# Attention's matrix powers and its inverse on TensorE: products that use the same weights joined to 128 columns, in quarters

## The chip, the cores and the metric

The kernel runs on one core of a Trainium2 chip. The metric is the device time of one execution in microseconds. A core has a matmul engine (TensorE, PE in the profile, with PEld for its weight loads), three engines for elementwise work (VectorE or DVE, ScalarE or ACT, GpSimd or POOL) and SyncE (SP), which issues DMAs. Matmul results land in PSUM, from which DVE and ACT copy them to SBUF. Each engine works through its own queue in order; semaphores tie them together.

## What is computed

The whole program is an attention with a state per head, then a mixture of experts, then a feed-forward layer. The change is in the attention alone:

```python
batch, n_heads, seq, head_dim = (4, 8, 768, 40)
for t in range(S):
    y[:, :, t] = np.einsum('bhd,bhde->bhe', rt, state)
    Sa = np.einsum('bhde,bhe->bhd', state, at)
    state_decay = state * wt[:, :, None, :] - np.einsum('bhd,bhe->bhde', Sa, bt)
    state = state_decay + np.einsum('bhd,bhe->bhde', vt, kt)
```

The 768 steps are cut into 12 chunks of 64. Inside a chunk the dependence of a step on the earlier ones is a triangular 64x64 matrix, whose inverse the kernel builds; from chunk to chunk a state is carried.

## The kernel before

`attention` handles the 32 heads in 8 groups of 4, each with 12 chunks, so a "wide" product covers a half of the chunks (6) for four heads: 24 matmuls of 64x64x64, written as `square` (L365). The inverse of `I + N` is a product of `I + N^(2^k)`: `n2`, `n4`, `n8`, `n16` are powers of N, `t2`, `t4`, `t8` the same powers of its transpose (a power of one kind takes the other as weights, so both are kept), and `w2`, `w4`, `w8`, `w16` multiply the inverse so far, `wb`, by `n2`, `n4`, ... and add. `_0` and `_1` are the halves. Note that `t4` and `w2` both load `n2` as weights, and `t8` and `w4` both load `n4`.

Each wide product goes into one of three PSUM slots (`wide0` to `wide2`), by its number modulo 3. Product n may start when product n-3 has been taken:

```python
if n >= 3 and kind != "Y":
    taken(pe, *in_order[n - 3])
```

`n`, `t`, `K`, `B`, `V`, `L`, `UT`, `ST` and `X` are taken by ACT (`BY_ACT`), the others by DVE. `w` products are added to `wb` by DVE (L641).

Alongside runs the recurrence over the chunks of the group before, in hops `u`, `s`, `r`: a small product on PE, then a copy of it on ACT (`u`, L553), the state on DVE (`s`, L681) or the right-hand side on DVE (`r`, L674), and the next hop waits for that.

The order is written out by hand. One table, `ORDER`, holds the tokens of a turn of the loop (a turn prepares one group and runs the recurrence of the one before); PE, ACT and DVE each walk through the same table and do their share, in that order. `LEAD` is the table of the first turn (turn 0), which has no recurrence, and turns 1 to 7 use `ORDER`. `p0` and `p1` are tokens of DVE alone: `make_decays` (L661) for the next group, with two scans (L664, L667) and two short steps, in turns 0 to 6. GpSimd rounds N, starts `wb` (L352), subtracts the identity (L356), and scales the operands of the next group.

Of the kernel before, what the change touches and what calls it, by code (L numbers as in the profile page):

```python
# [27 lines left out]
P = 128  # L28
# [8 lines left out]

ORDER = """u ST1 N0 s UT1 T0 r N1 u H1 I1 t2_0 s J1 Y1 r T1 u n2_0 s t2_1 r w2_0 u K1 s n2_1 r t4_0 u p0 t4_1 K0 n4_1 s  # L40
n4_0 M0 B0 r w4_0 u w2_1 ST0 s M1 r UT0 w4_1 u n8_0 s t8_1 r n8_1 u t8_0 V1 p1 s n16_1 n16_0 w8_0 X1 r H0 u
w16_0 s w8_1 I0 r E0 B1 u w16_1 L0 s V0 r E1 u J0 s Y0 L1 r F0 X0 F1 u""".split()

LEAD = """N0 K1 N1 K0 T0 M1 T1 n2_0 M0 n2_1 B0 t2_0 t2_1 w2_1 n4_0 w2_0 B1 n4_1 p0 t4_1 t4_0 V1 n8_0 w4_0 t8_1 t8_0 p1
w8_0 n8_1 n16_0 w4_1 n16_1 w16_0 w8_1 V0 L0 w16_1 E0 E1 L1 F0 F1""".split()
DRAIN = """u s ST1 r u s r u UT1 s r H1 u s r u s r u s r u s I1 r J1 Y1 u UT0 s r H0 u X1 s r u ST0 s I0 r J0 Y0 u s
X0 r u""".split()
CHAIN = ("u", "s", "r")
FIRST_HALF = ("UT0", "ST0", "H0", "I0", "J0", "Y0", "X0")
SECOND_HALF = ("ST1", "UT1", "H1", "I1", "J1", "Y1", "X1")  # L50
BY_ACT = ("n2", "n4", "n8", "n16", "t2", "t4", "t8", "K", "B", "V", "L", "UT", "ST", "X")


def split(tok):
# [10 lines left out]
def attention(nc, wdec, at, kb, vt, vd, rb, rc, gate_w, x, logits, ident):  # L65

    GR, _, D, _, S = at.shape
    C = 64
# [21 lines left out]
    for it in range(GR + 2):  # L90
        for tok in order_of(it):
            g = group_of(tok, it)
            if g is None or tok in CHAIN or tok[0] in "Jp":
                continue
            by = "act" if split(tok)[0] in BY_ACT else "dve"
            ends[by] += 1
            number[tok, g] = len(number)
            count[tok, g] = by, ends[by]
    in_order = list(number)

    def chunk_of(hop):
# [3 lines left out]
    with ExitStack() as ctx:  # L105
# [24 lines left out]
        tpow = [sb(f"tpow{b}", [P, 2, S], BF16) for b in range(2)]  # L130
        wb = sb("wb", [P, 2, S], BF16)
# [31 lines left out]

        def taken(eng, tok, g):

            by, n = count[tok, g]
            eng.wait_ge(act_done if by == "act" else dve_done, n)

        def cells():

# [193 lines left out]
        def _(pe):  # L364
# [8 lines left out]
            def wide(tok, g):  # L373
# [29 lines left out]
                elif kind[0] in "nt":  # L403
                    p = int(kind[1:])
                    at_ = (p.bit_length()) % 2
                    if p == 2:
                        pe.wait_ge(rounded, 2 * g + half + 1)
                        taken(pe, f"T{half}", g)
                    else:
                        taken(pe, f"n{p // 2}_{half}", g)  # L410
                        taken(pe, f"t{p // 2}_{half}", g)
                    left, right = (tpow, npow) if kind[0] == "n" else (npow, tpow)
                    m = square(half, out, left[at_], right[at_])
                elif kind[0] == "w":
                    p = int(kind[1:])
                    taken(pe, f"n{p}_{half}", g)
                    if p == 2:
                        pe.wait_ge(started, 2 * g + half + 1)
                    else:
                        taken(pe, f"w{p // 2}_{half}", g)  # L420
# [130 lines left out]
        def _(act):  # L551
# [3 lines left out]
            def take(tok, g):  # L555
# [6 lines left out]
                if kind[0] in "nt":  # L562
                    p = int(kind[1:])
                    dst = (npow if kind[0] == "n" else tpow)[(p.bit_length() + 1) % 2]
                    if kind == "t4":
                        act.wait_ge(started, 2 * g + half + 1)
                    m = copy(dst[:, :, at_], t[:, :, 0:W])
                elif kind in ("K", "B"):
                    m = copy(kbtok[b2][:, 0 if kind == "K" else 1, half * HC:half * HC + HC].rearrange("q (b c) h d -> q b (c h) d", b=2),
                             t[:, :, 0:W].rearrange("q b (n f) -> q b n f", f=C)[:, :, :, 0:D])  # L570
# [23 lines left out]
            for it in range(GR + 2):  # L594
                hop = 0
                for tok in order_of(it):
# [3 lines left out]
                    if tok in CHAIN:  # L600
# [8 lines left out]
                        elif kind == "r" and c < NC - 1:  # L609
# [4 lines left out]
                    elif tok[0] not in "Jp" and split(tok)[0] in BY_ACT:  # L614
                        take(tok, g)
                    elif tok in ("w16_0", "w16_1"):
                        half = split(tok)[1]
                        taken(act, tok, g)
                        copy(wb[:, :, cols(half, W)], w0[g % 2][:, :, cols(half, W)]).then_inc(w_rounded, 1)

        @block.vector
        def _(dve):
# [3 lines left out]
            def take(tok, g):  # L626
# [771 lines left out]
```

## Time and profile before

| | us |
|---|---|
| median of 3 runs | 1591.04 (1590.13 to 1598.68) |
| profiled execution | 1593.16 |
| its span, first to last instruction | 1591.4 |
| PE busy | 1440.8 (91%) |
| DVE busy | 578.8 (36%) |
| ACT busy | 587.5 (37%) |
| GpSimd busy | 293.0 (18%) |

Times are those of one profiled execution. An engine's queue is read from top to bottom: when its next instruction waits, all behind it wait. Attention lies between about 28 and 576 us. The timeline merges instructions of a line that follow each other; "x24" with 0.57 us is a product of 24 matmuls from its first start to its last end. A matmul of a float32 operand stands as two instructions.

### The profile page before, as it was taken

Reading aid. Unit: us, or ns where it says so; the run is one execution under the profiler, and the core shown is the slowest. Engines: PE = TensorE matmul, PEld = TensorE weight load, DVE = VectorE, ACT = ScalarE, POOL = GpSimd, SP = SyncE. Lnnn points to the kernel's source line nnn. Section 1 sums busy time; section 2 is a strip of 40 time slices with the busy share of each in tenths; the row PEclk is TensorE's granted clock in tenths of the full one; section 3 lists DMA queues with packets and bytes.
Section 4 is the critical chain, followed back from the end, with each engine's and each line's share of the span. In section 5 each row is a group of like instructions: output and inputs, shape, how many; then the busy total and the mean of one; then the engine's idle time right before and its main releaser. Section 6 shows DMA issues by size and latency. Waiting matters only on the chain.

```text
span 1591.4 us, 45341 instructions
## 1 busy us (share of the span) xinstructions
PE 1440.8 (91%) x19945; PEld 1115.7 (70%) x19945; DVE 578.8 (36%) x1107; ACT 587.5 (37%) x1167; POOL 293.0 (18%) x263
## 2 busy tenths in 40 slices
PE   2889989899898727999999999999699999999999
PEld 2778878788787626888888888888435555555556
DVE  6665565564643260000000000000165445445441
ACT  1555364453544321111211112111176545554451
POOL 5532233232220001111111111111320010000000
PEclk9787797876878657999999999999799999999999
DMA  3223232222311177555555555556410011000000
GB/s 117 61 87 94 68 105 74 80 82 73 92 44 35 52 228 248 185 170 172 168 181 183 170 170 168 185 178 203 128 50 21 26 32 31 25 17 9 13 9 21
DMA packets 87553, 161.20 MB, mean 101 GB/s; under 512 B 39552, under 2 KB 53888, under 8 KB 87360
## 3 DMA queue, kind: packets, MB, share of 16 engines
q1 hardware_dynamic: 79776, 132.41, 26.5%
q0 software_dynamic: 7584, 25.90, 5.3%
q8 instruction: 160, 2.62, 0.7%
q14 instruction: 33, 0.27, 0.1%
HBM read 141.39 MB, written 16.88 MB: 99 GB/s over the span
## 4 chain that ended last, share of the span: by engine, by line
PE 60%; DMA 1%; issue 1%; DVE 0%; ACT 0%; POOL 0%; POOLq 0%; DVEq 0%
PE pY L1027 15%; PE pY L1169 13%; PE pH L1008 13%; PE pH L1156 11%; PE pH L1013 4%; PE pH L1159 3%; PE pX L997 1%; PE pX L1144 1%; PE pX L998 0%; DMA xs<-x,slot_token 0%; DMA rows<-results,pos 0%; POOL rows L1135 0%; DVE down L1244 0%; DMA results<-ys 0%; ACT mxT L1198 0%
## 5 line engine op out<-in xcount | busy, mean ns | idle before, releaser
L1027 PE MATMUL pY<-down,hT 128*128 x880 | 245.9, 433 | 0.0
L1008 PEld LDWEIGHTS pH<-exT,up 128*128 128x128 f32 x1760 | 207.9, 194 | 11.5 <-issue 1.7
L1053 ACT ACTIVATE hT<-pH 128x512 f32<-128x512 f32 x110 | 59.7, 594 | 419.4 <-PE pH L1013 419.4
L1061 DVE COPY ys<-pY 128x320 f32<-128x320 f32 x55 | 27.0, 492 | 507.1 <-PE pY L1027 507.1
L1008 PE MATMUL pH<-exT,up 128*128 128x128 f32 x1760 | 208.5, 277 | 2.5 <-ACT exT L1046 2.5
L1169 PE MATMUL pY<-wout,down 128*128 128x320 f32 x768 | 210.4, 433 | 0.0
L1027 PEld LDWEIGHTS pY<-down,hT 128*128 128x128 f32 x880 | 163.0, 190 | 61.2
L1169 PEld LDWEIGHTS pY<-wout,down 128*128 128x128 f32 x768 | 144.3, 190 | 60.7 <-issue 3.0
L1156 PE MATMUL pH<-mxT,win 128*128 128x512 f32 x384 | 172.5, 603 | 4.9 <-ACT mxT L1198 4.7
L1156 PEld LDWEIGHTS pH<-mxT,win 128*128 128x128 f32 x384 | 73.8, 193 | 91.6 <-issue 82.2
L988 POOL DMA_DIRECT2D results<-ys x55 | 31.9, 580 | 428.4 <-DVE ys L1061 428.4
L1135 POOL DMA_INDIRECT rows<-results,pos x48 | 45.7, 952 | 221.4 <-DVE mix L1223 209.9
L1206 ACT ACTIVATE down<-down 128x512 f32<-128x512 f32 x64 | 39.9, 629 | 122.0 <-DVE down L1244 122.0
L553 ACT ACTIVATE npow<-wide 128x768 bf16<-128x768 f32 x80 | 63.3, 811 | 39.6 <-PE wide L427 23.1
L553 ACT ACTIVATE uv<-chain 64x80 f32<-64x80 f32 x192 | 44.3, 231 | 84.6 <-PE chain L525 82.9
L1235 DVE TENSOR_TENSOR down<-down 128x512 f32<-128x512 f32 x64 | 40.0, 686 | 94.6 <-ACT down L1212 94.5
L1245 DVE COPY down<-pH 128x512 f32<-128x512 f32 x96 | 65.2, 679 | 0.0
L1013 PE MATMUL pH<-exT,up_rest 64*128 64x128 f32 x880 | 63.9, 285 | 0.0
L202 POOL TENSOR_TENSOR kbT<-kbT,after 128x1536 f32<-128x1536 f32 x15 | 51.6, 3444 | 62.5 <-DMA kbT<-in_kb 62.5
L979 POOL DMA_INDIRECT xs<-x,slot_token x55 | 53.8, 978 | 49.8 <-POOLq L732 30.1
L525 PE MATMUL chain<-rhs,w 64*64 64x40 f32 x768 | 49.1, 250 | 10.7 <-DVE rhs L674 5.0
L1244 DVE TENSOR_SCALAR down<-pH 128x512 f32<-128x512 f32 x64 | 43.7, 683 | 39.8 <-PE pH L1159 31.0
(189 smaller groups left out, 2146.0 us busy)
## 6 DMA issues: line engine op xcount, KB each, us to landing
up<-in_moe_w SPq DMA_DIRECT2D x55, 1024.0 KB, 5.2
up_rest<-in_moe_w SPq DMA_DIRECT2D x110, 128.0 KB, 5.1
down<-in_moe_w SPq DMA_DIRECT2D x8, 1280.0 KB, 14.3
results<-ys POOLq DMA_DIRECT2D x55, 160.0 KB
wfr<-in_wdec SPq DMA_DIRECT2D x32, 240.0 KB
kbT<-in_kb SPq DMA_DIRECT2D x32, 240.0 KB
uv<-in_vt SPq DMA_DIRECT2D x16, 312.0 KB, 3.8
aT<-in_at SPq DMA_DIRECT2D x16, 240.0 KB
```

What stands on the lines that cost most here:

```text
L202: unit.tensor_tensor(kbT[:, i], kbT[:, i], backwards, ALU.mult).then_inc(kb_scaled, 1)
L525: m = pe.matmul(chain[x:x + 64, h, 64:64 + D], w0[b2][x:x + 64, h, cols(c, C)], rhs[b2][x:x + 64, h, c, :], start=True, stop=True)
L553: return nc.scalar.activation(out, in_, ACT.Copy, scale=scale)
L979: nc.gpsimd.indirect_dma_start(out=xs[t % 3][:], out_offset=None, in_=x, in_offset=bass.IndirectOffsetOnAxis(ap=slot_token[:, t:t + 1], ax ...
L1008: pe.matmul(pH[t % 2][b][:, c, :], up[t % NU][:, k, f * P:(f + 1) * P], xT[t % 2][:, k, :], start=(c == 0 and k == 0), stop=False, skip_gr ...
L1013: m = pe.matmul(pH[t % 2][b][:, c, :], up_rest[t % NU][at, c * P:(c + 1) * P], xT[t % 2][at, 2, :], start=False, stop=True, skip_group_che ...
L1027: m = pe.matmul(pY[t % 2][:, 0:D], hT[t % 2][:, j, :], down[:, bass.ds(e, 1), j, :].rearrange("q n d -> q (n d)"), start=(j == 0), stop=(j ...
L1053: nc.scalar.activation(hT[t % 2][:, b * HT:(b + 1) * HT, :], pH[t % 2][b][:], ACT.Relu).then_inc(h_copied[b], 1)
L1156: pe.matmul(pH[f % 4], win[:, k, f * P:(f + 1) * P], xT[g % 2][:, k, :], start=(k == 0), stop=False)
L1159: pe.matmul(pH[f % 4], win_rest[at, f // 2 * P:(f // 2 + 1) * P], xT[g % 2][at, 2, :], start=False, stop=True).then_inc(h_done, 1)
L1169: m = pe.matmul(pY[t % 2][:, 0:D], h[g % 2][:, f, j * P:(j + 1) * P], wout[:, f, :], start=(f == 0), stop=(f == FT - 1))
L1245: nc.vector.tensor_copy(h[g % 2][:, GT * q + f, :], pH[f]).then_inc(h_used, 1)
```

## The change

`t4` and `w2` become `q4`, `t8` and `w4` become `q8`. A `q` product loads a block of `n2` (or `n4`) once and multiplies it by 128 columns, 64 of `t` and 64 of `wb`, which therefore lie in one tensor `tw`. Its results have twice the columns, so one slot holds a quarter of the chunks: `q4_0` to `q4_3` and `q8_0` to `q8_3` replace the eight half products, in eight places of the tables that these had. A quarter is 12 matmuls. ACT copies its `t` part and then DVE adds its `w` part; a slot is free when both are through. `q` products therefore stand in the queues of both ACT and DVE.

```diff
-ORDER = """u ST1 N0 s UT1 T0 r N1 u H1 I1 t2_0 s J1 Y1 r T1 u n2_0 s t2_1 r w2_0 u K1 s n2_1 r t4_0 u p0 t4_1 K0 n4_1 s
-n4_0 M0 B0 r w4_0 u w2_1 ST0 s M1 r UT0 w4_1 u n8_0 s t8_1 r n8_1 u t8_0 V1 p1 s n16_1 n16_0 w8_0 X1 r H0 u
+ORDER = """u ST1 N0 s UT1 T0 r N1 u H1 I1 t2_0 s J1 Y1 r T1 u n2_0 s t2_1 r q4_0 u K1 s n2_1 r q4_1 u p0 q4_2 K0 n4_1 s
+n4_0 M0 B0 r q8_0 u q4_3 ST0 s M1 r UT0 q8_2 u n8_0 s q8_3 r n8_1 u q8_1 V1 p1 s n16_1 n16_0 w8_0 X1 r H0 u
...
-LEAD = """N0 K1 N1 K0 T0 M1 T1 n2_0 M0 n2_1 B0 t2_0 t2_1 w2_1 n4_0 w2_0 B1 n4_1 p0 t4_1 t4_0 V1 n8_0 w4_0 t8_1 t8_0 p1
-w8_0 n8_1 n16_0 w4_1 n16_1 w16_0 w8_1 V0 L0 w16_1 E0 E1 L1 F0 F1""".split()
+LEAD = """N0 K1 N1 K0 T0 M1 T1 n2_0 M0 n2_1 B0 t2_0 t2_1 q4_2 n4_0 q4_0 B1 n4_1 p0 q4_3 q4_1 V1 n8_0 q8_0 q8_2 q8_1 q8_3
+p1 w8_0 n8_1 n16_0 n16_1 w16_0 w8_1 V0 L0 w16_1 E0 E1 L1 F0 F1""".split()
...
-BY_ACT = ("n2", "n4", "n8", "n16", "t2", "t4", "t8", "K", "B", "V", "L", "UT", "ST", "X")
+BY_ACT = ("n2", "n4", "n8", "n16", "t2", "K", "B", "V", "L", "UT", "ST", "X")
...
+        def together(kind):
+
+            return (1, 1, 0) if kind == "q4" else (0, 0, 1)
...
+                elif kind[0] == "q":
+
+                    p = int(kind[1:]) // 2
+                    taken(pe, f"n{p}_{half // 2}", g)
+                    if p == 2:
+                        taken(pe, f"t2_{half // 2}", g)
+                        pe.wait_ge(started, 2 * g + half // 2 + 1)
+                    else:
+                        taken(pe, f"q4_{half}", g)
+                    lo = together(kind)[0]
+                    for c in range(HC // 2):
+                        k = half * (HC // 2) + c
+                        for i, h, e, x, z in cells():
+                            m = pe.matmul(out[x:x + 64, h, cols(c, 2 * C)], npow[(p.bit_length() + 1) % 2][x:x + 64, h, cols(k, C)],
+                                          tw[x:x + 64, lo:lo + 2, h, cols(k, C)], start=True, stop=True)
...
+                elif kind[0] == "q":
+                    if kind == "q4":
+                        act.wait_ge(started, 2 * g + half // 2 + 1)
+                    m = copy(by_chunk(tpow[0 if kind == "q4" else 1][:, :, cols(half, W // 2)]),
+                             t[:, :, 0:W].rearrange("q h (c s f) -> q h c s f", s=2, f=C)[:, :, :, together(kind)[1], :])
...
-                elif kind in ("w2", "w4", "w8"):
+                elif kind[0] == "q":
+
+                    dve.wait_ge(act_done, count[tok, g][0][1])
+                    part = by_chunk(wb[:, :, cols(half, W // 2)])
+                    m = nc.vector.tensor_tensor(part, t.rearrange("q h (c s f) -> q h c s f", s=2, f=C)[:, :, :, together(kind)[2], :], part, ALU.add)
+                elif kind == "w8":
```

DVE's queue around `p0` in turn 1 (`p0` is the four rows from `after` to `dec_0`; `wb` or `tw` with 192 is a `w` add, `st` the state of hop `s`, `rhs` that of hop `r`, `mT` is `M0`). Before:

```order
L674 TENSOR_TENSOR rhs<-chain,rhs 128x2x40
L664 SCALAR_TENSOR_TENSOR after<-wfr,mark_r 128x768
L665 TENSOR_TENSOR fend<-after,wfr 128x12
L666 RECIPROCAL mark<-fend 128x12
L667 SCALAR_TENSOR_TENSOR dec_0<-wfr,mark 128x768
L681 SCALAR_TENSOR_TENSOR st<-chain,fend,fs 128x40 x2
L639 TENSOR_TENSOR mT<-wide,mask_u 128x2x384
```

Now, in the same place:

```order
L711 TENSOR_TENSOR rhs<-chain,rhs 128x2x40
L676 TENSOR_TENSOR tw<-wide,tw 128x2x192
L701 SCALAR_TENSOR_TENSOR after<-wfr,mark_r 128x768
L702 TENSOR_TENSOR fend<-after,wfr 128x12
L703 RECIPROCAL mark<-fend 128x12
L704 SCALAR_TENSOR_TENSOR dec_0<-wfr,mark 128x768
L676 TENSOR_TENSOR tw<-wide,tw 128x2x192
L718 SCALAR_TENSOR_TENSOR st<-chain,fend,fs 128x40 x2
L671 TENSOR_TENSOR mT<-wide,mask_u 128x2x384
```

An add (of `q4_1`) now stands ahead of `p0`, and one (of `q4_2`) between `p0` and the state.

PE's queue in the same place, from `t4_1` to `w4_0`, with the slot's number in `wide0` to `wide2`. Before:

```order
L369 MATMUL wide0<-tpow1,npow1 64x64 x24
L395 MATMUL wide1<-ident,kbT 128x128 x6
L369 MATMUL wide2<-npow1,tpow1 64x64 x24
L532 MATMUL chain<-uv0,kbtok0 40x40 x4
L369 MATMUL wide0<-npow1,tpow1 64x64 x24
L390 MATMUL wide1<-aT1,kbT 64x64 x24
L395 MATMUL wide2<-ident,kbT 128x128 x6
L514 MATMUL chain<-st,aT0 64x40 x4
L369 MATMUL wide0<-wb,npow0 64x64 x24
```

Now:

```order
L441 MATMUL wide0<-tw,npow1 64x128 x12
L406 MATMUL wide1<-ident,kbT 128x128 x6
L380 MATMUL wide2<-npow1,tw 64x64 x24
L561 MATMUL chain<-uv0,kbtok0 40x40 x4
L380 MATMUL wide0<-npow1,tw 64x64 x24
L401 MATMUL wide1<-aT1,kbT 64x64 x24
L406 MATMUL wide2<-ident,kbT 128x128 x6
L543 MATMUL chain<-st,aT0 64x40 x4
L441 MATMUL wide0<-tw,npow0 64x128 x12
```

Nothing moved here; the first row, which is `q4_2` now, and the fifth, `n4_0`, share slot `wide0` as `t4_1` and `n4_0` did, and the first is now freed by ACT and DVE instead of ACT alone.

DVE's queue around `p1` in turn 1 (the four rows from `after` to `dec_1`). Before:

```order
L641 TENSOR_TENSOR wb<-wide,wb 128x2x384
L681 SCALAR_TENSOR_TENSOR st<-chain,fend,fs 128x40 x2
L674 TENSOR_TENSOR rhs<-chain,rhs 128x2x40
L664 SCALAR_TENSOR_TENSOR after<-wfr,mark_r 128x768
L665 TENSOR_TENSOR fend<-after,wfr 128x12
L666 RECIPROCAL mark<-fend 128x12
L667 SCALAR_TENSOR_TENSOR dec_1<-wfr,mark 128x768
L681 SCALAR_TENSOR_TENSOR st<-chain,fend,fs 128x40 x2
L641 TENSOR_TENSOR wb<-wide,wb 128x2x384
```

Now:

```order
L676 TENSOR_TENSOR tw<-wide,tw 128x2x192
L718 SCALAR_TENSOR_TENSOR st<-chain,fend,fs 128x40 x2
L676 TENSOR_TENSOR tw<-wide,tw 128x2x192
L711 TENSOR_TENSOR rhs<-chain,rhs 128x2x40
L676 TENSOR_TENSOR tw<-wide,tw 128x2x192
L701 SCALAR_TENSOR_TENSOR after<-wfr,mark_r 128x768
L702 TENSOR_TENSOR fend<-after,wfr 128x12
L703 RECIPROCAL mark<-fend 128x12
L704 SCALAR_TENSOR_TENSOR dec_1<-wfr,mark 128x768
L718 SCALAR_TENSOR_TENSOR st<-chain,fend,fs 128x40 x2
L678 TENSOR_TENSOR tw<-wide,tw 128x2x384
```

The adds of `q8_3` and `q8_1` are new, one ahead of hop `r`'s step and one ahead of `p1`.

## Rows read from the trace of the kernel before

**Rows 1.** The page's first lines: span, busy time and share of each engine.
```profile
span 1591.4 us, 45341 instructions
PE 1440.8 (91%) x19945; PEld 1115.7 (70%) x19945; DVE 578.8 (36%) x1107; ACT 587.5 (37%) x1167; POOL 293.0 (18%) x263
```

**Rows 2.** Attention's stretch: PE, PEld, DVE, ACT, POOL busy, granted clock, DMA share, GB/s.
```profile
60.00:560.00 500.00, 442.89 (x13867) 399.24 (x13866) 269.76 (x498) 237.18 (x618) 126.28 (x68) 0.79 0.26 73
```

**Rows 3.** PE's waits in that stretch: us in total, times, longest.
```profile
PE chain L532 <- ACT uv L553: 8.1, 24, 0.7
...
PE wide L369 <- issue: 5.6, 7, 1.9
PE wide L434 <- issue: 5.4, 7, 2.2
```

**Rows 4.** Timeline of turn 3, DVE's `p0` and what follows; ACT's taking of `t4_0`.
```profile
207.62 2.93 DVE L664 TENSOR_TENSOR_SCAN after<-wfr,mark_r 128x768 f32<-128x768 f32 x1
...
211.06 1.76 DVE L667 TENSOR_TENSOR_SCAN dec<-wfr,mark 128x768 f32<-128x768 f32 x1
212.73 0.40 DVE L681 SCALAR_TENSOR_TENSOR st<-chain,fend,fs 128x40 f32<-128x40 f32 x2
...
208.23 0.80 ACT L553 ACTIVATE tpow<-wide 128x768 bf16<-128x768 f32 x1
```

**Rows 5.** Timeline of turn 3, PE: `t4_1`, `s`, `n4_0`, `B0`, `r`.
```profile
208.01 0.61 PE L369 MATMUL wide<-tpow,npow 64*64 64x64 bf16 x24
...
209.85 0.35 PE L532 MATMUL chain<-uv,kbtok 128*40 128x40 f32 x8
210.27 0.57 PE L369 MATMUL wide<-npow,tpow 64*64 64x64 bf16 x24
...
211.59 0.88 PE L395 MATMUL wide<-ident,kbT 128*128 128x128 f32 x6
213.19 0.33 PE L514 MATMUL chain<-st,aT 40*64 40x40 f32 x8 [0.72 <-DVE st L681]
```

**Rows 6.** Groups by shape: takes of 384 and of 768 elements a partition.
```profile
L553 ACT ACTIVATE uvT<-wide 104x384 f32<-104x384 f32 x32 | 13.9, 488 | 20.2 <-PE wide L447 20.2
...
L650 DVE TENSOR_TENSOR yT<-wide,dec 128x384 f32<-128x384 f32 x32 | 16.4, 553 | 41.4 <-PE wide L485 41.4
...
L553 ACT ACTIVATE tpow<-wide 128x768 bf16<-128x768 f32 x48 | 38.5, 809 | 22.1 <-PE wide L369 21.3
...
L641 DVE TENSOR_TENSOR wb<-wide,wb 128x768 bf16<-128x768 f32 x48 | 45.7, 954 | 18.5 <-PE wide L369 17.4
```

**Rows 7.** Timeline of turn 3: GpSimd's subtraction, and DVE from `p1` on.
```profile
205.35 3.58 POOL L356 TENSOR_TENSOR n<-n,eye 128x768 f32<-128x768 f32 x2
...
220.61 1.75 DVE L664 TENSOR_TENSOR_SCAN after<-wfr,mark_r 128x768 f32<-128x768 f32 x1
...
224.54 0.40 DVE L681 SCALAR_TENSOR_TENSOR st<-chain,fend,fs 128x40 f32<-128x40 f32 x2
225.91 0.96 DVE L641 TENSOR_TENSOR wb<-wide,wb 128x768 bf16<-128x768 f32 x1 [0.97 <-PE wide L369]
228.55 0.24 DVE L674 TENSOR_TENSOR rhs<-chain,rhs 128x80 f32<-128x80 f32 x1 [1.68 <-PE chain L514]
```

**Rows 8.** Timeline of turn 3, ACT: the copy of hop `u` after `UT0`, and `t8_0`.
```profile
218.57 0.47 ACT L553 ACTIVATE uv<-chain 64x80 f32<-64x80 f32 x2
...
222.99 0.81 ACT L553 ACTIVATE tpow<-wide 128x768 bf16<-128x768 f32 x1
```

**Rows 9.** The lead: DVE's `p0` and `w8_0`, PE's `w4_1`, then a window (columns as rows 2).
```profile
45.80 1.75 DVE L664 TENSOR_TENSOR_SCAN after<-wfr,mark_r 128x768 f32<-128x768 f32 x1
...
55.57 0.93 DVE L641 TENSOR_TENSOR wb<-wide,wb 128x768 bf16<-128x768 f32 x1
56.55 0.85 PE L369 MATMUL wide<-wb,npow 64*64 64x64 bf16 x24 [3.42 <-DVE wb L641]
...
56.50:66.00 9.50, 9.39 (x333) 9.27 (x334) 5.31 (x6) 4.09 (x6) 7.93 (x3) 0.50 0.01 3
```

**Rows 10.** The page's row on the queue that brings instructions: packets, MB, share.
```profile
q8 instruction: 160, 2.62, 0.7%
```

More of the change, by code:

```diff
@@ L94, in attention @@
                 continue
-            by = "act" if split(tok)[0] in BY_ACT else "dve"
-            ends[by] += 1
             number[tok, g] = len(number)
-            count[tok, g] = by, ends[by]
+            count[tok, g] = []
+            for by in ("act", "dve") if tok[0] == "q" else ("act",) if split(tok)[0] in BY_ACT else ("dve",):
+                ends[by] += 1
+                count[tok, g].append((by, ends[by]))
     in_order = list(number)
@@ L129, in attention @@
         npow = [sb(f"npow{b}", [P, 2, S], BF16) for b in range(2)]
-        tpow = [sb(f"tpow{b}", [P, 2, S], BF16) for b in range(2)]
-        wb = sb("wb", [P, 2, S], BF16)
+        tw = sb("tw", [P, 3, 2, S], BF16)
+        tpow, wb = [tw[:, 0], tw[:, 2]], tw[:, 1]
         w0 = [sb(f"w0{b}", [P, 2, S]) for b in range(2)]
@@ L164, in taken, with taken_half @@
         def taken(eng, tok, g):
-            by, n = count[tok, g]
-            eng.wait_ge(act_done if by == "act" else dve_done, n)
+            for by, n in count[tok, g]:
+                eng.wait_ge(act_done if by == "act" else dve_done, n)
+        def taken_half(eng, kind, half, g):
+            for quarter in (2 * half, 2 * half + 1):
+                taken(eng, f"{kind}_{quarter}", g)
+        def together(kind):
+            return (1, 1, 0) if kind == "q4" else (0, 0, 1)
         def cells():
@@ L410, in wide @@
                         taken(pe, f"n{p // 2}_{half}", g)
-                        taken(pe, f"t{p // 2}_{half}", g)
+                        if p == 4:
+                            taken(pe, f"t2_{half}", g)
+                        else:
+                            taken_half(pe, f"q{p // 2}", half, g)
                     left, right = (tpow, npow) if kind[0] == "n" else (npow, tpow)
                     m = square(half, out, left[at_], right[at_])
+                elif kind[0] == "q":
[4 more added lines that the diff above has]
+                        pe.wait_ge(started, 2 * g + half // 2 + 1)
+                    else:
+                        taken(pe, f"q4_{half}", g)
[5 more added lines that the diff above has]
+                                          tw[x:x + 64, lo:lo + 2, h, cols(k, C)], start=True, stop=True)
                 elif kind[0] == "w":
@@ L416, in wide @@
                     taken(pe, f"n{p}_{half}", g)
-                    if p == 2:
-                        pe.wait_ge(started, 2 * g + half + 1)
+                    if p == 8:
+                        taken_half(pe, "q8", half, g)
                     else:
-                        taken(pe, f"w{p // 2}_{half}", g)
+                        taken(pe, f"w8_{half}", g)
                     m = square(half, out, npow[(p.bit_length() + 1) % 2], wb)
@@ L564, in take @@
                     dst = (npow if kind[0] == "n" else tpow)[(p.bit_length() + 1) % 2]
-                    if kind == "t4":
-                        act.wait_ge(started, 2 * g + half + 1)
                     m = copy(dst[:, :, at_], t[:, :, 0:W])
+                elif kind[0] == "q":
[3 more added lines that the diff above has]
+                             t[:, :, 0:W].rearrange("q h (c s f) -> q h c s f", s=2, f=C)[:, :, :, together(kind)[1], :])
                 elif kind in ("K", "B"):
@@ L613, in _ @@
                             m.then_inc(fs_ready, 1)
-                    elif tok[0] not in "Jp" and split(tok)[0] in BY_ACT:
+                    elif tok[0] == "q" or tok[0] not in "Jp" and split(tok)[0] in BY_ACT:
                         take(tok, g)
```

## The prediction

> **What bounds the kernel now.** I read the page first: TensorE (PE) is busy 91% of a span of 1591.4 us [rows 1]. The change touches only attention, some 560 us of it, so the next view is the busy time of that stretch: from 60 to 560 us PE is busy for 442.9 of 500 us at a mean granted clock of 0.79 [rows 2]. PE takes its work in one fixed order, so what counts is where PE stands still, and the view of who waited for whom tells that: its idle time is many short waits, on the recurrence's copies (8.1 us in 24 waits, none over 0.7) and on nothing the profile shows ("issue": 5.6 us before the squares and 5.4 before another line, up to 2.2 us each) [rows 3]. No wait is long because each thing that PE needs is taken off early enough. The question is whether the new order of takers keeps that.
>
> The timeline of one steady turn (turn 3 of the loop) shows the place where it is tight. At 207.62 VectorE (DVE) starts `p0`, the decays of the next group: a scan of 2.93 us, two short steps and a scan of 1.76 us. Its next work, the state of hop `s`, starts at 212.73 [rows 4]. For 5.1 us nothing that DVE takes from PSUM is taken. Yet PE runs on through `t4_1`, `K0`, `n4_1`, `s`, `n4_0`, `M0` and `B0` and idles only 0.72 us, before hop `r` at 213.19 [rows 5], because `t4_1`, `K0`, `n4_1` and `n4_0` are all taken by ScalarE (ACT).
>
> **The change part by part.**
>
> *The product.* A half product of 24 matmuls at the full clock lasts 0.57 us [rows 5]; less the 0.19 us of the last one, 16.5 ns from one to the next. They alternate between two halves of the array, so each half spends 33 ns on 64 columns, which are 26.7 ns at 2.4 GHz: 6.3 ns are not columns. No row shows a bf16 product of 64 rows with 128 columns. Joining a `t` half and a `w` half takes 24 loads away. If a matmul of 128 columns keeps one such 6.3 ns, the pair saves 12 x 6.3 = 0.075 us; if it keeps none, 0.15 us. Below these, nothing is saved: in the lead, at 1.2 GHz, the product of 24 took 0.85 us [rows 9], 26.5 ns each or 53 per half of the array, which is 64 columns and nothing else. I take 0.11 us x 4 pairs x 8 groups = 3.5 us at the full clock, and as PE often waits there anyway, -2 us.
>
> *A rule against this.* The row says 33 ns per 64 columns in each half of the array. The Trainium skill (TensorE: Matmul & The Clock Gate, Back-to-back issue gap) gives about 60 cycles for a matmul of up to 64 columns and 134 for one of 128, so a joined matmul would be longer than two small ones, by 14 cycles. By that a joined pair of products would cost 0.07 us more, and the term would be +2 us and not -2. The trace disagrees at 64 columns (33 ns against 25), which is where the saving would come from.
>
> *The instruction stream.* 768 matmuls and 768 weight loads go, of 13867 + 13866 in the 500 us [rows 2], 5.5%. The kernel's stream came in 160 blocks [rows 10]. If the stream's arrival set PE's pace everywhere, 5.5% of 500 us, 27 us, would go; if it set none, nothing. The "issue" waits say it sets some: eleven rows of that kind hold about 25 us, and 5.6 us stand before the squares [rows 3]. I take -1 us per turn, -7 us, and keep 0 and -20 for the range. The trace has waits of up to 2.2 us for nothing shown, on a stream that doesn't branch. The Trainium skill (Runtime: NRT & Kernel Launch, Instruction fetch mechanics) says that crossing a block is mostly hidden; by it this term would be 0 and the sum 7 us higher.
>
> *The takers.* Before, a product has one taker: 0.81 us on ACT or 0.95 us on DVE. A quarter now has two, one after the other, since DVE waits for ACT. No row shows 128x384 taken with this pattern; the nearest are 0.49 us on ACT and 0.55 us on DVE [rows 6]. So a slot is held 0.49 + 0.05 + 0.55 = 1.1 us. The engines have room (270 and 237 us busy of 500, [rows 2]); what matters is who stands in line.
>
> *p0, the main term.* `q4_1` stands where `t4_0` stood, but DVE must take it before it starts `p0`. ACT took `t4_0` at 208.23 [rows 4]; so DVE is through with `q4_1` at 208.23 + 1.1 = 209.3 and starts `p0` 1.7 us later than now. Part comes back: the first scan took 2.93 us beside GpSimd's subtraction, which lasts to 208.93, against 1.75 us in `p1`, where the whole block of decays lasted 3.9 us [rows 4, 7]. So `p0` now ends at 213.3. Behind it on DVE stands `q4_2`, which PE fills just before `K0`, and its add ends at 213.8. Three products later `n4_0` writes the same slot, and PE may not start it before that. It started at 210.27; `M0`, `B0` and all after it stand behind it in PE's queue. From `n4_0` to the end of `B0` are 2.2 us [rows 5]; hop `r` then starts at 213.85 + 2.2 = 216.05 instead of 213.19: +2.9 us per turn. It holds in the six turns that have a `p0` (1 to 6): +17.4 us. The wait of PE before `n4_0` is 3.4 us.
>
> *p1.* DVE must now also take `q8_3` and `q8_1` before `p1`. ACT took `t8_0` at 222.99 [rows 8], so `p1` starts at 224.1 instead of 220.61 and ends at 228.0; the state of hop `s` and the add of `w8_0`, 0.95 us, follow and end at 229.4 instead of 226.87. Hop `r`'s DVE step, now at 228.55, comes behind them [rows 7]: up to 0.9 us late. I take +0.6 us in six turns, +3.6 us.
>
> *Steps that now stand in line before the recurrence.* On ACT, `q4_0` and `q8_2` are new in front of the copy of hop `u` (the copy after `w4_1` started at 218.57, right behind another take, [rows 8]): up to 0.49 us each. On DVE `q8_3` is new in front of hop `r`. I take 1.0 us in seven turns, +7 us, with 0 and 10 as ends.
>
> *The lead.* The same two blocks stand in group 0. `p0` starts at 45.80; with `q4_0` taken first it starts at about 46.6 and ends at 50.6. `q4_3` is behind it, and `n8_0` waits for its slot and for `q4_1`. Then `n8_0` and four quarters must be taken, about 5 us, before `p1` runs from 55.9 to 59.9, and `w8_0` is added at 60.8 instead of 56.50, the end that PE now waits 3.42 us for [rows 9]. One product of 0.65 us no longer stands behind it: +3.7 us.
>
> *The clock.* After that wait of 3.42 us PE's granted clock was 0.50 for the next 9.5 us [rows 9]. The new wait of every turn is as long. A product costs 0.28 us more at 1.2 GHz (0.85 against 0.57). If the clock is low for some 4 us of work per turn, that is 1.5 us: +9 us for six turns. Ends: 0, and 48 us (16 us low per turn).
>
> **Sum:** 17.4 + 3.6 + 7 + 3.7 + 9 - 2 - 7 = +31.7 us on the profiled execution's 1593.2 us, 1624.9. That execution lies 2.1 us above the median of 1591.0, so the median of after should be 1623.
>
> **The rivals.**
>
> *Faster: the stream decides.* If PE's pace is set by the arrival of its instructions, 27 us go with the removed ones, and the new waits let the stream run ahead and give back most of what they cost, some 20 us. For it: the "issue" waits. Against it: they are 25 us in all, and around 208 us there is none. It decides if they exceed 3 us per turn before `n4_0`. The costs of the sum are 40.7 us; less the clock's 9 and 20 of waits given back they are 11.7: 1591 - 27 + 11.7 = 1576.
>
> *No change: absorbed.* The wait before `n4_0` stands, but nearly all later idle of the turn (issue and copies, about 4 us per turn) vanishes, since PE comes later to each: 31.7 - 25 = +7 us, 1598. Against it: the copies' waits follow PE's own products and shift with them.
>
> *Slower by more: the clock.* If a wait of 3.4 us drops the clock for 16 us rather than 4, six turns lose 48 us instead of 9: 1662. For it: 9.5 us low after the only such wait. Against it: in the steady turns the work behind it is dense.
>
> *The order isn't what it seems.* If the quarter behind `p0` had its add elsewhere, the terms of p0, the lead and the clock would go, 31.7 - 17.4 - 3.7 - 9 = +1.6 us, 1593. The built program's order on DVE shows it behind `p0`.
>
> **How the numbers follow.** Forecast 0.70; stream decides 0.05; absorbed 0.06; clock 0.16; order 0.03. The forecast's own bounds: down 18 us (stream -20, line 0, some clock), up 25 us. The range reaches part of the way to the clock's case: 1603 to 1650. Over 0.5% (8 us), which is about what a measurement can tell from no change: faster 0.05, same 0.06 and slower 0.89.
>
> **What would show it.** In the timeline of after, PE should idle some 3.4 us before the 24 matmuls of `n4_0`, released by DVE's add of a quarter that follows the scans; the first scan of `p0` should be near 1.75 us; hop `r` should follow 2.2 us later. The wait for DVE's add should lead PE's list of waits with about 20 us. Quarters should take 0.49 and 0.55 us. I am wrong if PE doesn't idle at `n4_0`, if the "issue" waits fall by over 15 us, or if the clock's mean in the 500 us stays at 0.79 or rises.

## The result, and the profile after

| | before | after |
|---|---|---|
| median, us | 1591.17 (1590.13 to 1598.68) | 1624.39 (1617.97 to 1628.82, 4 runs) |
| profiled execution, us | 1593.16 | 1628.82 |
| its span, us | 1591.4 | 1627.0 |

The ratio is 1.0182 with a 95% interval of [1.0155, 1.0209]: slower by 29 us (24.7 to 33.3). The medians differ by 33 us. The prediction said 1623. The profiled execution is the slowest of its four.

The page's first lines answer [rows 1], and its row on the instruction queue [rows 10] (160 blocks before). TensorE has 768 matmuls fewer and is busy as long as before.

```profile
span 1627.0 us, 44138 instructions
...
PE 1441.3 (89%) x19177; PEld 1114.3 (68%) x19177; DVE 577.9 (36%) x1139; ACT 591.6 (36%) x1199; POOL 292.4 (18%) x263
...
q8 instruction: 155, 2.54, 0.7%
```

The busy time from 60 to 560 us (columns as [rows 2]) shows 24 us less of PE's work done in the same 500 us. The mean clock is 0.80, not below the 0.79 of before.

```profile
60.00:560.00 500.00, 418.77 (x12571) 376.10 (x12571) 260.20 (x500) 232.06 (x613) 129.52 (x69) 0.80 0.26 70
```

PE's waits from 60 to 600 us (us in total, times, longest) answer [rows 3]. The first row had 5.6 us before and now has 21.6, and its longest is 3.5. The next rows are little changed in total (7.6 for 5.4, 7.1 for 8.1; the last had 5.7 us in 11 waits, the longest 0.7).

```profile
PE wide L380 <- issue: 21.6, 7, 3.5
PE wide L463 <- issue: 7.6, 7, 1.8
...
PE chain L561 <- ACT uv L582: 7.1, 21, 0.7
PE chain L543 <- DVE st L718: 6.9, 9, 2.7
```

The place of the loss is in the timeline of turn 3, which answers [rows 4] and [rows 5]. First VectorE (DVE): the add of `q4_1`, the four instructions of `p0`, the add of `q4_2`, and the state of hop `s`.

```profile
225.55 0.56 DVE L676 TENSOR_TENSOR tw<-wide,tw 128x384 bf16<-128x384 f32 x1 [1.10 <-ACT tw L582]
226.03 1.75 DVE L701 TENSOR_TENSOR_SCAN after<-wfr,mark_r 128x768 f32<-128x768 f32 x1
...
228.29 1.76 DVE L704 TENSOR_TENSOR_SCAN dec<-wfr,mark 128x768 f32<-128x768 f32 x1
...
229.96 0.53 DVE L676 TENSOR_TENSOR tw<-wide,tw 128x384 bf16<-128x384 f32 x1
...
230.41 0.41 DVE L718 SCALAR_TENSOR_TENSOR st<-chain,fend,fs 128x40 f32<-128x40 f32 x2
```

Then ScalarE (ACT), which had taken its half of `q4_2` 4 us earlier, and PE: hop `s`, the wait, `n4_0`, `B0`, hop `r`.

```profile
225.83 0.49 ACT L582 ACTIVATE tw<-wide 128x384 bf16<-128x384 f32 x1
...
226.71 0.35 PE L561 MATMUL chain<-uv,kbtok 128*40 128x40 f32 x8
...
230.59 0.47 PE L380 MATMUL wide<-npow,tw 64*64 64x64 bf16 x19 [3.53 <-issue]
...
232.36 1.54 PE L406 MATMUL wide<-ident,kbT 128*128 128x128 f32 x6
...
233.83 0.45 PE L543 MATMUL chain<-st,aT 40*64 40x40 f32 x8
```

PE stands still from 227.06 to 230.59 and starts again 0.1 us after DVE's add has ended. The profile calls this "issue", which is what it says when it finds no releaser; the semaphore that `n4_0` waits for is still that of the add, since the slot is the one of `q4_2`. Each of turns 1 to 6 has this wait, 3.53 us long. Behind it the clock is low, from 0.6 us after PE's start at the latest. The columns of the next rows are again those of [rows 2]; they are the wait and the 6.75 us behind it.

```profile
226.00:230.55 4.55, 0.93 (x33) 0.72 (x32) 4.45 (x7) 1.59 (x3) 0.36 (x1) 1.00 0.38 99
230.55:237.30 6.75, 6.71 (x127) 5.79 (x129) 2.59 (x6) 3.21 (x9) 1.45 (x1) 0.54 0.15 45
```

In the lead, [rows 9] are answered by `w8_0`'s add, which ends at 59.83 (before: 56.50), and two long waits where there was one:

```profile
50.27 0.85 PE L380 MATMUL wide<-npow,tw 64*64 64x64 bf16 x24 [2.06 <-DVE tw L676]
...
58.90 0.93 DVE L678 TENSOR_TENSOR tw<-wide,tw 128x768 bf16<-128x768 f32 x1
...
59.89 0.85 PE L380 MATMUL wide<-npow,tw 64*64 64x64 bf16 x24 [4.11 <-DVE tw L678]
```

To compare the kernels place by place, I cut each steady turn at PE's starts of hops and products. The table has the mean over turns 1 to 6 of the profiled execution, in us with the granted clock; "rest" is the remainder of the turn. The hops are numbered by the chunk that they work for, so hop r 5 comes just before hop u 5. The clocks are plain means of the six turns. Each kernel has one profiled execution, so differences of a few tenths mean little. Two of the six executions of `e10_p0_alone`, the profiled one among them, ran in a slower state (1634 us) and count neither here nor in its ratio.

| kernel | hop u 3 to n4_0 | n4_0 to hop r 5 | r 5 to u 7 | u 7 to r 8 | rest | turn |
|---|---|---|---|---|---|---|
| before | 5.29 @.99 | 2.95 @.96 | 8.65 @.90 | 7.51 @.85 | 38.50 | 62.90 |
| after | 9.16 @.93 | 3.47 @.53 | 8.82 @.86 | 8.34 @.86 | 38.78 | 68.58 |
| e1_p0_behind_q4_2 | 5.65 @.97 | 4.20 @.99 | 10.45 @.66 | 7.03 @.92 | 39.29 | 66.64 |
| e2_t4_by_dve | 8.76 @.92 | 3.42 @.55 | 8.18 @.88 | 8.30 @.82 | 38.95 | 67.62 |
| e3_two_loads | 9.30 @.92 | 3.58 @.51 | 8.80 @.87 | 8.46 @.86 | 38.39 | 68.54 |
| e4_filled_wait | 13.04 @.96 | 2.03 @1.0 | 8.22 @1.0 | 7.74 @.83 | 38.83 | 69.87 |
| e5_short_fill | 9.24 @.97 | 2.03 @1.0 | 8.23 @1.0 | 7.36 @.87 | 39.45 | 66.32 |
| e6_after_split_decays | 5.72 @.94 | 2.55 @1.0 | 9.32 @.97 | 8.23 @.71 | 38.42 | 64.25 |
| e7_before_split_decays | 5.32 @.99 | 2.32 @1.0 | 8.46 @.96 | 7.39 @.91 | 38.58 | 62.06 |
| e8_before_no_decays | 5.40 @1.0 | 2.25 @1.0 | 7.80 @1.0 | 7.69 @.89 | 38.90 | 62.05 |
| e9_after_no_decays | 5.61 @.98 | 2.03 @1.0 | 8.79 @1.0 | 7.14 @.94 | 37.84 | 61.41 |
| e11_p1_alone | 5.54 @.99 | 2.03 @1.0 | 8.69 @1.0 | 7.90 @.90 | 37.96 | 62.12 |
| e12_decays_in_gaps | 5.95 @.89 | 2.03 @1.0 | 8.45 @1.0 | 7.02 @.96 | 49.00 | 72.45 |

From before to after the turn grows by 5.7 us, of which 3.9 lie ahead of `n4_0`.

### The profile page after: what moved, and what is told of

Its sections match the earlier page's. It is cut to its first block, busy times and chain, and to the rows that moved or that the text cites. A ratio compares the mean times of both kernels' runs of the same rounds, so it can differ in the third digit from the quotient of the medians.

```text
span 1627.0 us, 44138 instructions
## 1 busy us (share of the span) xinstructions
PE 1441.3 (89%) x19177; PEld 1114.3 (68%) x19177; DVE 577.9 (36%) x1139; ACT 591.6 (36%) x1199; POOL 292.4 (18%) x263
## 4 chain that ended last, share of the span: by engine, by line
PE 58%; DMA 1%; issue 1%; DVE 0%; ACT 0%; SPq 0%; POOL 0%; POOLq 0%; DVEq 0%
PE pY L1064 14%; PE pY L1206 13%; PE pH L1045 12%; PE pH L1193 10%; PE pH L1050 4%; PE pH L1196 3%; PE pX L1034 1%; PE pX L1181 1%; DMA up_rest<-in_moe_w 0%; PE pX L1035 0%; DVE down L1281 0%; DMA rows<-results,pos 0%; DVE down L1282 0%; DMA results<-ys 0%; ACT mxT L1235 0%
## 5 line engine op out<-in xcount | busy, mean ns | idle before, releaser
L380 PE MATMUL wide<-npow,tw 64*64 64x64 bf16 x1536 | 38.7, 200 | 30.9 <-issue 22.7
```

## The experiments

Theory A, that of the prediction: the loss comes from the decays standing on DVE between takers that PE waits for, above all `p0` ahead of the add of `q4_2`, and from the low clock behind that wait. Theory B: the low clock is the larger part. Theory C: the quarters with their two takers cost wherever they stand. (In the first expectation below, "Theory B" is something else: that the wait only moves.) The kernel before ran beside each group of kernels, and ratios are to its runs there.

**`p0` moved behind `q4_2`.**

```diff
-ORDER = """... r q4_1 u p0 q4_2 K0 n4_1 s
+ORDER = """... r q4_1 u q4_2 p0 K0 n4_1 s
```

> The changed kernel with one token moved in the table of the steady turns: p0, DVE's decays, stands behind q4_2 instead of ahead of it, so the slot of q4_2 is free before the decays begin. The lead's table is unchanged. Theory A (the slot behind p0): PE no longer stands still for 3.5 us before n4_0 in turns 1 to 6; what is late next is the state of hop s, some 0.5 us later than in the changed kernel, so hop r starts about 2.4 us earlier than there. Time 15 to 20 us below the changed kernel, about 1606. Theory B (the wait only moves to hop r, since the decays still hold the state): the wait before n4_0 goes and one of the same length appears before hop r, time within 5 us of the changed kernel's 1624.

It took 1623.17 us, ratio 1.0168 [1.0125, 1.0211], where theory A had 1606: that expectation failed, and the other outcome that it named came. The wait before `n4_0` is gone (hop u 3 to `n4_0` takes 5.65 us), but only 1.9 us per turn are gained. `p0` still stands ahead of the state of hop `s`, so an idle time of 2.1 us, in place of the 3.5, now stands before hop `r`, and the low clock behind it (timeline of turn 3, then the window behind the wait):

```profile
222.14 1.75 DVE L701 TENSOR_TENSOR_SCAN after<-wfr,mark_r 128x768 f32<-128x768 f32 x1
...
226.07 0.40 DVE L718 SCALAR_TENSOR_TENSOR st<-chain,fend,fs 128x40 f32<-128x40 f32 x2
...
226.53 0.45 PE L543 MATMUL chain<-st,aT 40*64 40x40 f32 x8 [2.10 <-DVE st L718]
```

```profile
226.50:237.50 11.00, 10.26 (x217) 9.00 (x217) 5.32 (x13) 6.90 (x19) 1.61 (x1) 0.56 0.33 94
```

So the product's slot was only the first that the block of 4 us delayed.

**`t4` taken by DVE in the kernel before**, so that `t4_1`'s taking stands behind `p0`; products and halves stay as they were.

```diff
-BY_ACT = ("n2", "n4", "n8", "n16", "t2", "t4", "t8", ...
+BY_ACT = ("n2", "n4", "n8", "n16", "t2", "t8", ...
+                elif kind == "t4":
+                    dve.wait_ge(started, 2 * g + half + 1)
+                    m = nc.vector.tensor_copy(tpow[0][:, :, at_], t)
```

> The kernel before with one thing changed: DVE takes t4_0 and t4_1 instead of ACT. No joined products, no quarters, no second taker. It puts a take ahead of p0 and one behind it, as the change does. Theory A (order of takers around p0 is most of the loss): PE waits 3 to 4 us before n4_0 in turns 1 to 6 and the time rises by 18 to 28 us over before, 1609 to 1619. Theory C (the loss is from the quarters and their two takers in a row): under 8 us over before.

It took 1621.87 us, ratio 1.0154 [1.0112, 1.0196], a loss of 24.5 us. With no joined product and no quarter the same wait, with the same low clock behind it (3.42 us at 0.55), brings a loss of nearly the same size, and here the profile names what ended it:

```profile
PE wide L369 <- DVE tpow L640: 20.9, 6, 3.6
```

**Each matmul of 128 columns as two of 64**, each with its load, in the changed kernel; slots, takers and order unchanged.

```diff
-                            m = pe.matmul(out[x:x + 64, h, cols(c, 2 * C)], ..., tw[x:x + 64, lo:lo + 2, h, cols(k, C)], ...)
+                            for s in range(2):
+                                m = pe.matmul(out[x:x + 64, h, cols(2 * c + s, C)], ..., tw[x:x + 64, lo + s, h, cols(k, C)], ...)
```

> The changed kernel with each joined matmul of 128 columns cut into two of 64 with a weight load each: same places, same takers, same slots, but the 768 matmuls and weight loads are back. It prices the joined product alone. By the prediction's terms (2 us of columns and 7 us of instruction stream) it is 9 us slower than the changed kernel, 1633. If the 'issue' waits don't hang on the number of instructions and PE waits in these places anyway, it is within 3 us of 1624.

It took 1633.72 us, ratio 1.0238 [1.0201, 1.0276]: 0.0056 or 8.9 us above the changed kernel, uncertain by some 7. A quarter at the full clock, joined in the changed kernel (first row) and split here (second), and the groups of all quarters from 60 to 595 us, joined and split:

```profile
221.12 0.53 PE L441 MATMUL wide<-tw,npow 64*64 64x128 bf16 x12
```
```profile
225.22 0.57 PE L442 MATMUL wide<-tw,npow 64*64 64x64 bf16 x24
```
```profile
L441 PE MATMUL wide<-tw,npow 64*64 64x128 bf16 x672 | 33.1, 236 | 0.2 <-issue 0.2
```
```profile
L442 PE MATMUL wide<-tw,npow 64*64 64x64 bf16 x1344 | 36.8, 204 | 0.2
```

The join saves 0.04 us a quarter and 3.7 us of busy time in the 56 quarters of the stretch. At the low clock a quarter takes 0.86 us joined and 0.86 split. Turns 1 to 6 are equally long with it and without it (68.58 and 68.54 us), so what it saves there is eaten by the waits. The 8.9 us have no clear place either: of the 6.1 us between the spans of the two profiled executions 1.4 lie ahead of turn 1, 2.6 in turn 7 and the end of attention, and 2.3 behind attention, where the kernels are the same.

**The wait filled, twice.** Float32 matmuls into a free slot, their results unused, ahead of `n4_0` in turns 1 to 6: eleven of them (as shown), and five.

```diff
+                if tok == "n4_0" and 1 <= g < GR - 1:
+                    taken(pe, "K0", g)
+                    for _ in range(11):
+                        pe.matmul(slot[(n + 1) % 3][:, 0, 0:W], ident[:], mask_u[:].rearrange("q c f -> q (c f)"), start=True, stop=True)
```

> The changed kernel with work in the wait: in turns 1 to 6, ahead of n4_0, PE multiplies 11 times a constant 128x384 tile by the identity into the slot that M0 overwrites next (about 3.5 us, results unused). The slot's wait stays, PE's idle time there goes. Theory D (the clock after the wait costs what the prediction says): the granted clock stays 1.0 from n4_0 to hop r, this stretch takes 2.2 to 2.8 us instead of 3.2 to 3.6, and the time falls by 5 to 12 us against the changed kernel, to about 1615. Theory E (low stretches only come elsewhere, the mean clock of attention stays 0.79): within 3 us, or up to 5 us slower where the filling runs over the end of the wait.

> The changed kernel with five float32 matmuls put ahead of n4_0 in turns 1 to 6; they write a slot that is free then, and their results are used by nothing. At 0.64 us each they last 3.2 us and fit into the wait of 3.5 us, where e4's eleven overran it. Both theories have n4_0 start when DVE's add of q4_2 is through, as in the changed kernel. If the granted clock falls because PE stood idle, and that costs what e4's stretches showed (1.4 us from n4_0 to r5 and 0.6 us from r5 to u7), the six turns get back 12 us: about 1612 where the kernel before has 1593, the stretch from n4_0 to hop r 5 takes 2.0 us at a clock near 1.0 and not 3.5 at 0.53. If the low clock costs nothing in the end (it comes later in the turn instead), 1624.

Eleven took 1643.18 us, ratio 1.0309 [1.0249, 1.037]: they last 7.36 us, not the 3.5 that I had expected but twice the wait, so `n4_0` came 3.9 us later than in the changed kernel. Yet the clock stayed at 1.00 behind them. Five fit (timeline of turn 3 and the window behind the wait):

```profile
224.74 3.49 PE L391 MATMUL wide<-mask_u,ident 128*128 128x384 f32 x10
228.34 0.47 PE L380 MATMUL wide<-npow,tw 64*64 64x64 bf16 x19
```

```profile
228.30:238.60 10.30, 9.04 (x297) 7.62 (x297) 5.72 (x15) 7.78 (x21) 1.45 (x1) 1.00 0.38 102
```

That kernel took 1615.52 us, ratio 1.0126 [1.0072, 1.0181], 0.0056 or 8.9 us below the changed kernel, where 12 were expected. The intervals of the two overlap a little; what makes the reading firm is the stretch behind the wait, 2.03 us at 1.00 against 3.47 at 0.53, in the mean of six turns. By the runs the clock is 8.9 of 29 us, but uncertain by nearly 10. The traces say more: with the wait still there and the clock at 1.00 behind it, a turn is 2.3 us shorter than in the changed kernel (66.32 against 68.58), and still 3.4 us longer than before. So the clock is about two fifths of what a turn lost and the wait the larger part: theory B falls, by one trace of each kernel. Part of the gain is paid back elsewhere: the turn's first stretch, hop u 0 to u 3, became 1.1 us longer (19.22 at 0.59 against 18.16 at 0.69).

**The decays cut in two and moved**, in the changed kernel and in the kernel before. `p` is now the first scan and the two short steps, `d` the second scan; the lead is changed likewise.

```diff
-... q4_1 u p0 q4_2 K0 n4_1 s n4_0 M0 B0 r q8_0 ... w8_0 X1 r H0 u
+... q4_1 u q4_2 p0 K0 n4_1 s n4_0 M0 B0 r d0 q8_0 ... w8_0 d1 X1 r H0 u
```

> The changed kernel with DVE's decays cut in two and moved: the first scan and its two short steps (2.2 us) behind q4_2, the second scan (1.8 us) behind hop r; likewise for p1 (second scan behind w8_0) and in the lead, where the first part now stands behind q4_3 and q4_1. All the work is still done. Theory A (the place of the decays among the takers is the loss): no wait before n4_0, under 0.5 us before hop r, lead 2 us shorter than in the changed kernel; with the joined product's 9 us kept, the time is 25 to 38 us below the changed kernel, 1586 to 1599, level with or a little under before. Theory C (quarters with two takers cost by themselves): it stays over 1600.

> The kernel before with its decays cut in two in the same way, without joined products: what the cut alone is worth, as the control for the run beside it. The kernel before waits about 0.7 us at hop r in six turns and 3.4 us in the lead; I expect 3 to 8 us below before. If the joined product is worth its 9 us once nothing stands behind the decays, the run beside it is 0 to 9 us below this one; if the quarters' takers eat that, they are equal or this one is faster.

The changed kernel took 1601.55 us, ratio 1.0048 [1.0019, 1.0077]; the kernel before 1591.95, ratio 0.9996 [0.9968, 1.0025]. Moving and cutting the blocks alone takes back 21 us of the 29 in the changed kernel (1586 to 1599 had been expected, so it fell just short), and nothing that can be measured in the kernel before, where I had expected 3 to 8 us.

**No decays at all**, in both. For the groups after the first, the decays are those of the first group (copied once ahead of the loop), and `p0` and `p1` are one short memset, so their result isn't the reference's.

```diff
-                            make_decays(it + 1, int(tok[1]))
+                            dve.wait_ge(w_loaded[int(tok[1])], (it + 2) * 32)
+                            wait(dve, kb_scaled, 2 * (it + 1))
+                            nc.vector.memset(mark[:, int(tok[1])::C], 0.0).then_inc(decayed, 1)
```

> The kernel before without the decays of groups 1 to 7: group 0's are copied instead, and each later p0 and p1 is one short memset on DVE, so its output isn't the reference's. It takes the suspected cost away altogether. Theory A: 6 to 14 us below before (0.7 us and less at hop r, 3 us in the lead, some clock).

> The changed kernel without the decays of groups 1 to 7, in the same way (output not the reference's). With nothing long on DVE, what is left between this and the run beside it is joined products, quarters and second takers alone. Theory A: within 5 us of the kernel before without decays (9 us gained by the join, up to 7 lost to the takers in line), so 35 to 45 us below the changed kernel. Theory C (the quarters cost by themselves): over 10 us slower than the run beside it.

The kernel before took 1592.93 us, ratio 1.0015 [0.9993, 1.0037]; the changed one 1588.96, ratio 0.9987 [0.9955, 1.0019]. The 14 blocks of decays in the loop, some 4 us each on DVE, cost the kernel before nothing that can be measured (6 to 14 us had been expected), and the changed kernel all of its loss (0.0195 or 31 us). Theory C falls with this: without the decays the quarters with their two takers, the gain of the join included, are level with the halves. The add of `q4_2` ran from 209.73 to 210.29 there, and `n4_0` followed at 210.39 without a wait:

```profile
210.01 0.35 PE L561 MATMUL chain<-uv,kbtok 128*40 128x40 f32 x8
210.39 0.47 PE L380 MATMUL wide<-npow,tw 64*64 64x64 bf16 x19
```

**One block alone.** The changed kernel with `p0` kept in turns 1 to 6 and all other decays left out as above, and the same with `p1`.

```diff
-                        if it + 1 < GR:
+                        if it + 1 < GR and it > 0 and tok == "p0":
                             make_decays(it + 1, int(tok[1]))
```

> The changed kernel with p0 kept in turns 1 to 6, and p1 in those turns and both in the lead left out (a one-step memset in their place; the decays of the later groups are partly those of the first, so the result isn't the reference's). Without any decays it was 1589 where the kernel before had 1593. If p0 is the main term, as the sum has it (17.4 us and 9 of clock), about 1615; if the loss comes from p1 and the lead just as much, about 1604. The wait before n4_0 should stand as in the changed kernel, u3 to n4_0 9.2 us.

> The changed kernel with p1 kept in turns 1 to 6, and p0 in those turns and both in the lead left out, in the same way. The sum had p1 at 3.6 us: 1589 + 4 = 1593. If p1 is behind as much of the loss as p0 (the stretch from u7 to hop r 8 was 0.8 us longer and w8_0's slot late), 1604. What e10, e11 and the kernel without decays leave of the changed kernel's 1624 is the lead's part, or what they do to each other: 1 to 6 us.

`p0` alone: 1608.30 to 1619.49 us, ratio 1.0127 [1.0077, 1.0177]. `p1` alone: 1591.27 us, ratio 1.0003 [0.9972, 1.0034]. Above the 0.9987 without decays these are 22.3 us for `p0`, uncertain by some 9, and 2.5 us for `p1`, which by the runs can't be told from nothing.

**The pieces put into DVE's idle time**, everything computed: `p0` at the start of the turn, `p1` ahead of `Y1`, `d0` at `V1`, `d1` at `X1` (the reciprocal belongs to `d` here); the lead's table is changed likewise.

```diff
-ORDER = """u ST1 N0 s UT1 ... s J1 Y1 r T1 ... q4_1 u p0 q4_2 ... q8_1 V1 p1 s ... w8_0 X1
+ORDER = """u p0 ST1 N0 s UT1 ... s J1 p1 Y1 r T1 ... q4_1 u q4_2 ... q8_1 V1 d0 s ... w8_0 d1 X1
```

> The changed kernel with everything computed, the decays cut in two (p: scan and ends, 1.9 us; d: reciprocal and scan, 1.9 us) and each piece put where DVE stood idle in the trace without decays: p0 at the turn's start ahead of N0 (3.1 us idle), p1 ahead of Y1 (3.7), d0 at V1 (1.6), d1 at X1 (1.7). If the loss is the decays' place among the takers, this comes within 4 us of the kernel without decays: 1589 to 1594, where the kernel before has 1593. If decays anywhere delay a taker, or e6's 8 us came from the split itself, 1600 or more.

It took 1658.12 us, ratio 1.0421 [1.0373, 1.0469], and neither expectation saw why. I had looked at DVE's idle time and not at SyncE's queue. SyncE issues a group's load of decays after hop 1, and the second half after hop 6, of the very turn that uses them; a scan placed before that waits for the transfer, and the takers behind it wait too (waits of DVE, 60 to 600 us, then SyncE's issue and DVE's first scan in turn 3):

```profile
DVE after L706 <- DMA wfr<-in_wdec: 80.7, 12, 9.0
```

```profile
211.71 0.66 SPq L221 DMA_DIRECT2D wfr<-in_wdec  x2
...
217.76 1.76 DVE L706 TENSOR_TENSOR_SCAN after<-wfr,mark_r 128x768 f32<-128x768 f32 x1 [6.45 <-DMA wfr<-in_wdec]
```

Nearly the whole loss lies ahead of hop u 3, which comes 10.8 us later in the turn than without decays. From there on to hop r 8, where `d0` and `d1` stand, the stretches add up to what the kernel without decays has (5.95 + 2.03 + 8.45 + 7.02 = 23.5 us against 23.6). Earlier loads would be the next thing to try; that wasn't tried. No kernel that computes everything beat the kernel before, and the one without decays shows how little there is to win: 4 us below its counterpart, where the runs can tell some 6 apart.

## Why the prediction was right

The number was right to 1.4 us by the medians (1624.4 for 1623) and to 3 by the ratio (+29 for +31.7). The mechanism, `p0` ahead of an add that frees a slot, was right too. The terms behind it, as far as the runs price them (differences of ratios by 1591 us; each is uncertain by 4 to 14 us, most for `p0`'s wait and the lead's row):

| term | predicted | measured | from |
|---|---|---|---|
| p0, wait | +17.4 | +13.4 | `p0` alone less no decays, less the clock |
| the clock | +9 | +8.9 | changed less the fitting fill |
| p1 | +3.6 | +2.5 | `p1` alone less no decays |
| lead, and what the terms do to each other | +3.7 | +6.2 | the rest of the changed kernel |
| takers in line | +7 | +4.5 | no decays: changed less before (-4.4), plus the join |
| join and stream | -9 | -8.9 | two loads less changed |
| taking the decays from the kernel before | 0 | +2.4 | no decays, before |
| sum | +31.7 | +29.0 | |

The last column's differences add up to the measured one by construction, so their sum confirms nothing. Of the terms only the loss to `p0` as a whole (22.3 us, wait and clock together), the sum of all decays (31 us) and, barely, the join (8.9, uncertain by 7) are clear of nothing by the runs; the traces tell the others apart, with one execution each. That the sum came so close is in part luck: the takers in line at +7 and the stream at -7 cancel, and no run shows either by itself.

*p0.* Every step of the working is in the timeline: the first scan took 1.75 us, not 2.93; the adds took 0.56 and 0.53 us; the wait was 3.5 us for 3.4 (the working's own times, PE free at 210.20 and held to 213.85, give 3.6); it came in turns 1 to 6. The size is borne out better by the traces than by the table's 13.4. With the clock at 1.00 behind the wait (the five matmuls), hop u 3 to hop r 5 takes 11.27 us where it took 8.24 before: 3.0 us per turn for the 2.9 predicted, 18 us for 17.4. One number of the working was the end of a range: turn 3's scan of 2.93 us was the longest of the six before (2.14 to 2.93, in the mean 2.6), so a mean turn gets up to 0.3 us less back. Hop `r` followed after 3.24 us instead of 2.2, because the clock was low at once: `B0` took 1.54 us for 0.88. That difference belongs to the clock's term.

*p1 and the lead.* Hop u 7 to hop r 8 takes 7.90 us with `p1` alone and 7.14 without decays: 0.8 us per turn, 4.6 in six, for 3.6. The first hop of turn 1 starts at 67.3 us before, and at 68.9 to 72.8 us, 70.6 in the mean, in the five profiled kernels that share the changed kernel's lead: +3.3 us for +3.7. The 6.2 us in the table are this and what the terms do to each other.

*The clock.* The size was about right; the sign that I named for it was wrong. By the runs the term is 8.9 us, uncertain by nearly 10; by the turns of the traces it is 2.3 us each, 13.6 in six: `n4_0` to hop u 7 alone gives 2.0 (1.4 and 0.6). I had taken 1.5, for 4 us of work at the low clock, and the low stretch of turn 3 lasted 6.8 us. I had said that a mean of 0.79 or more would refute me. It was 0.80, and the term was there. The low stretch behind `n4_0` is real (0.54 for 6.75 us), but the wait ahead of it counts in turn 3's mean at 1.00, and the low stretch at the turn's start became shorter (hop u 0 to u 3 at 0.69 instead of 0.61). The window of 60 to 560 us also holds other parts of the loop in a slower kernel: over turns 1 to 6 the mean did fall, from 0.81 to 0.80, too little to be a sign of anything. The mean over a stretch weighs idle time like work. What should have been named is the clock of the one stretch behind the new wait.

*The instruction stream.* The sum's -9 for the join and the stream agrees with the end times of the two-loads kernel, but neither the split of it nor its place is shown. Of the 8.9 us, 3.7 are busy time of the products themselves (I took 3.5 at the full clock, and 2 in the sum); for the rest I argued from "issue" waits. These did not fall: all rows of that kind hold 53 us against 25 before (60 to 600 us), and less the six waits at `n4_0` still 32. The two-loads kernel, which has the 768 pairs back, has 44 us of them, and less the six waits 23: fewer, not more. Since the profile writes "issue" also where a semaphore held PE, the rows bear less than I put on them. No run shows a term of the stream, and what the remaining 5 us are stays open.

The Trainium skill (TensorE: Matmul & The Clock Gate, Back-to-back issue gap) would have a joined matmul last longer than two of 64 columns, by 14 cycles. The quarters disagree: 0.53 us joined and 0.57 us split, 12 matmuls against 24. The difference is in the price of 64 columns. Less the 0.22 us of its last matmul, a joined quarter has 28 ns from one matmul to the next, 56 ns in each half of the array for 128 columns, which agrees with the 134 cycles of the Trainium skill (56 ns at 2.4 GHz); the 33 ns for 64 columns are more than its 25.

*The wrong rivals.* "Stream decides" (1576) needed more than 3 us per turn of issue waits before `n4_0`. By its name in the profile such a wait is there, 3.5 us in each of six turns. But it ends 0.1 us behind DVE's add, goes when `p0` stands behind `q4_2`, and goes with the decays, with PE's instructions unchanged both times: it is the slot's. "Absorbed" (1598) needed later waits to vanish; PE's waits for ACT's `uv` are 7.1 us where they had 8.1. "Clock for 16 us" (1662) needed a longer low stretch; it was 6.8 us. Two figures beside the rivals were off in themselves. At the forecast's own rate of 1.5 us for 4 us, 16 us per turn would cost 36 us and not 48. And the rival on the order, at +1.6 us, belongs to "same", so the chances were 0.09 for same and 0.86 for slower.

## What to carry to other kernels

Before giving a buffer a second taker, look at what stands ahead of that taker in its queue: a block of 4 us on DVE was free while ScalarE freed the slots, and cost 22 us in the one place where an add behind it held one. Moving the block off one wait only uncovers the next thing behind it; cutting it in two as well, here and at `p1` and in the lead, took back 21 us where the move alone took back 2 (uncertain by 8). That this is because no piece then covers the time between two takers is my reading; no run varied the size of the pieces. And a gap in one engine's trace is free only if the data are there: check the queue that loads them.

## What the runs showed of the hardware

A wait of 3.5 us in which PE stood idle was followed by a granted clock of 0.54 over the next 6.75 us, and one of 2.1 us (`p0` moved behind `q4_2`) by 0.56 over the next 11. The wait of 3.5 us filled with ten float32 instructions of 0.35 us was followed by 10.3 us at 1.00. A load of the decays (two DMAs) was issued at 211.71 and let the scan start at 217.76, 6 us later. The first scan of `p0` took 2.14 to 2.93 us in the six turns of the kernel before in which GpSimd's subtraction (L356) ran beside it, and 1.75 us in all six of the changed kernel, where it did not.
